# Windowed attention ahead of a mixture of experts: 24 units in one order, scores on row halves, GpSimd normalises every half

## What is computed

```python
scores = (q @ k.T) / sqrt(64)                 # 4 batches, 8 heads, 576 tokens, 64 wide
mask_plain = (rel >= 0) & (rel < 32)          # heads 0 to 3
mask_dil = (rel >= 0) & (rel < 128) & (rel % 4 == 0)   # heads 4 to 7
attn = softmax(where(mask, scores, -1e9))
x = (attn @ v) as [2304 tokens, 512]
x = gate * expert(x)     # one of 8 experts per token, 512 -> 1024 -> 512, ReLU
out = softplus(x @ w_in) @ w_out              # 512 -> 2048 -> 512
```

## Time and profile before

| | us |
|---|---|
| median of 3 runs (813.33 to 814.98) | 814.34 |
| the profiled execution | 813.36 |
| its span, first to last instruction | 811.6 |

### The profile page before, as it was taken

How to read it: one execution, slowest core, us unless ns; L and a number is a source line. 1 busy time by engine, 2 the same in 40 slices (tenths; PEclk the granted TensorE clock), 3 DMA queues, 4 the chain that set the end, 5 groups by cost and what they waited for, 6 DMA issues and landing times.

```text
span 811.6 us, 14035 instructions
## 1 busy us (share of the span) xinstructions
PE 762.9 (94%) x4658; PEld 688.8 (85%) x4659; DVE 446.1 (55%) x910; ACT 398.4 (49%) x1014; POOL 235.2 (29%) x218
## 2 busy tenths in 40 slices
PE   5999996399999999999899999999999999999996
PEld 3667665289999999999899999999999989999995
DVE  8985986864665577767663343343334343334332
ACT  3995894034553566655563453353344344335332
POOL 6220220544666559777830010010010001001001
PEclk9999998589999999999999999999999999999999
DMA  9677202354654666775400010000000000001000
GB/s 247 182 186 271 115 0 117 90 166 152 215 176 136 200 206 192 232 217 181 132 26 1 1 39 0 0 39 0 0 26 13 0 0 39 0 0 39 0 0 39
DMA packets 27258, 74.55 MB, mean 92 GB/s; under 512 B 4112, under 2 KB 12320, under 8 KB 26720
## 3 DMA queue, kind: packets, MB, share of 16 engines
q1 hardware_dynamic: 20624, 53.52, 21.1%
q0 software_dynamic: 5744, 16.02, 6.7%
q10 hardware_dynamic: 864, 4.72, 1.5%
HBM read 64.79 MB, written 9.45 MB: 91 GB/s over the span
## 4 chain that ended last, share of the span: by engine, by line
PE 88%; DVE 7%; issue 2%; ACT 2%; POOL 0%; DVEq 0%; ACTq 0%
PE bank L620 13%; PE bank L622 13%; PE bank L621 13%; PE bank L644 8%; PE bank L646 8%; PE bank L642 8%; PE bank L633 4%; PE bank L635 4%; PE bank L634 4%; PE bank L499 4%; PE bank L523 2%; PE bank L536 2%; PE bank L509 2%; PE bank L606 1%; ACT probs L761 1%
## 5 line engine op out<-in xcount | busy, mean ns | idle before, releaser
L1237 DVE SCALAR_TENSOR_TENSOR g_sb<-bank,soft 128x384 f32<-128x384 f32 x96 | 53.6, 558 | 235.0 <-ACT soft L908 235.0
L904 ACT ACTIVATE soft<-bank 128x384 f32<-128x384 f32 x96 | 47.3, 492 | 208.7 <-PE bank L622 208.7
L471 POOL DMA_INDIRECT out<-y_sb,out_rows_i x18 | 17.5, 971 | 374.9 <-ACT y_sb L915 371.2
L1099 DVE TENSOR_TENSOR w_lo<-raw,w_hi 128x1024 fp32r<-128x1024 f32 x68 | 93.6, 1378 | 50.5 <-ACT w_hi L824 50.4
L620 PE MATMUL bank<-x_parts,w_hi 128*128 (+1 forms) x352 | 111.8, 318 | 3.7 <-DVE w_lo L1099 2.5
L622 PE MATMUL bank<-x_parts,w_lo 128*128 (+1 forms) x352 | 110.9, 315 | 0.0
L621 PE MATMUL bank<-x_parts,w_hi 128*128 (+1 forms) x352 | 110.8, 315 | 0.0
L824 ACT ACTIVATE w_hi<-raw 128x1024 fp32r<-128x1024 f32 x68 | 71.8, 1058 | 50.4 <-PE bank L635 49.6
L406 POOL TENSOR_SCALAR xs_sb<-landing,row_scale 128x256 f32<-128x256 f32 x48 | 64.3, 1348 | 65.8 <-PE bank L606 65.7
L633 PE MATMUL bank<-h_hi,w_hi 128*128 128x384 f32 (+3 forms) x256 | 80.7, 315 | 1.9 <-DVE h_lo L1119 1.9
L761 ACT ACTIVATE probs<-bank,neg_max 96x128 f32<-96x128 f32 x192 | 67.4, 366 | 22.5 <-DVE neg_max L950 22.5
(11 more groups left out here) (201 smaller groups left out, 1776.8 us busy)
## 6 DMA issues: line engine op xcount, KB each, us to landing
raw<-we SPq DMA_DIRECT2D x64, 512.0 KB, 3.5
x_tokens<-x_sb ACTq DMA_DIRECT2D x6, 768.0 KB, 5.1
v_sb<-vw SPq DMA_DIRECT2D x4, 1024.0 KB, 13.6
raw_m<-wm POOLq DMA_DIRECT2D x8, 512.0 KB, 5.2
raw<-wm SPq DMA_DIRECT2D x8, 512.0 KB, 3.6
q_sb<-qT SPq DMA_DIRECT2D x4, 768.0 KB, 9.1
k_sb<-kT SPq DMA_DIRECT2D x8, 384.0 KB, 11.4
v_sb<-vw SPq DMA_DIRECT2D x4, 512.0 KB, 4.7
```

Of the source, the lines that this page charges most:

```text
L1099: nc.vector.tensor_tensor(w_lo[:, r, :], raw[:, r, :], w_hi[:, r, :].bitcast(F32), ALU.subtract).then_inc(w_lo_done, 1)
```

## The change

One stream over all 24 units replaces the two turns; no counters, no turn boundary.

- **Scores on row halves.** A unit's eight heads are scored by eight matmuls of 64 rows and 128 columns. The even heads of the pairs (rows 0 to 63, `par` 0) go to one bank, the odd ones (rows 64 to 127, `par` 1) to the other, in turn. `k_sb` loses its zeros and their memsets, and a key load is one transfer. A bank now holds two plain and two dilated heads.
- **GpSimd normalises both halves** of each unit, one after the other, after one pair of small VectorE operations for the unit (`inverses`).
- **VectorE copies both transposed halves**; ScalarE none.
- **Token tiles between units.** Tiles 0 to 12 are done in units 8 to 11, 14 to 18 and 20 to 23, tiles 13 to 17 after the last unit.
- **Constants.** VectorE clears the masks and spreads the two large index tables from small ones; GpSimd loses those fills. Stores of tiles use three semaphores in turn.

```diff
-        k_sb = [sb(early, f"k_sb{s}", [P, PAIRS, 2, S]) for s in range(2)]
+        k_sb = [sb(early, f"k_sb{s}", [P, PAIRS, S]) for s in range(2)]
...
+        TILE_OF_UNIT = {}
+        for b_, tiles in enumerate((range(0, 4), range(4, 9), range(9, 13))):
+            for n_, g_ in enumerate(tiles):
+                TILE_OF_UNIT[UNITS * (b_ + 1) + 2 + n_] = g_
+        LATE_TILES = range(13, NT)
...
-                for par in range(2):
-                    r = slice(D * par, D * (par + 1))
-                    sp.dma_start(k_sb[m][r, :, par, lo:hi], kT[b][r, :, lo:hi]).then_inc(loaded, 16)
+                sp.dma_start(k_sb[m][:, :, lo:hi], kT[b][:, :, lo:hi]).then_inc(loaded, 16)
...
+            for n in range(2 * ALL_UNITS):
+                c = n % BANKS
+                pool.wait_ge(inv_ready, n // 2 + 1)
+                nc.gpsimd.tensor_tensor(probs[:, c, :, :], probs[:, c, :, :],
+                                        inv_sum[:, c, :].unsqueeze(2).to_broadcast([QT, HEADS, KEYS]), ALU.mult
+                                        ).then_inc(normed[n % 2], 1)
...
+            def scores(u):
...
+                if i == 2:
+                    pe.wait_ge(rest_loaded[m], 48 * (b // 2 + 1))
...
+                for par in range(2):
+                    if u > 1:
+                        pe.wait_ge(exps_done, 2 * (u - 2) + par + 1)
+                    if g is not None:
+                        pe.wait_ge(x_copied_dve if par else x_copied_act, g + 1)
+                    nc.tensor.matmul(banks[par][0:QT, :], identb[:, :], mask, start=True, stop=False,
+                                     skip_group_check=True)
+                for c in range(HEADS):
+                    for par in range(2):
+                        r = slice(D * par, D * (par + 1))
+                        last = nc.tensor.matmul(banks[par][0:QT, KEYS * c:KEYS * (c + 1)],
+                                                q_sb[m][r, c, q0:q0 + QT], k_sb[m][r, c, k0:k0 + KEYS],
+                                                start=False, stop=(c == HEADS - 1), skip_group_check=True)
+                        if c == HEADS - 1:
+                            last.then_inc(scores_done, 1)
...
+            for u in range(ALL_UNITS):
+                g = TILE_OF_UNIT.get(u)
+                if g is not None:
...
+                    pe.wait_ge(exps_done, 2 * u + 2)
+                    token_tile(g)
+                elif u + 2 < ALL_UNITS:
+                    scores(u + 2)
+                if u:
+                    values(u - 1)
+                for par in range(2):
+                    transposes(2 * u + par)
+                if g is not None and u + 2 < ALL_UNITS:
+                    scores(u + 2)
+            values(ALL_UNITS - 1)
+            for g in LATE_TILES:
+                pe.wait_ge(x_copied_act, g - 1)
+                pe.wait_ge(x_copied_dve, g - 1)
+                token_tile(g)
...
+            for u in range(ALL_UNITS):
+                g = TILE_OF_UNIT.get(u)
+                if u + 1 < ALL_UNITS:
+                    exps(2 * u + 2)
+                if g is not None:
+                    x_copy(g)
+                if u + 1 < ALL_UNITS:
+                    exps(2 * u + 3)
+                if u:
+                    dilated_tokens(u - 1)
+                if g is not None and g % TILES_STORED == TILES_STORED - 1:
+                    x_store(g)
...
-                for par in range(2):
-                    nc.vector.memset(k_sb[s][D * par:D * (par + 1), :, 1 - par, :], 0.0).then_inc(k_zeroed[s], 1)
...
+            def inverses(u):
+                pair = slice(2 * (u % 2), 2 * (u % 2) + 2)
+                dve.wait_ge(exps_done, 2 * u + 2)
+                nc.vector.tensor_scalar(sum_eps[:, pair, :], row_sum[:, pair, :], 1e-9, None, ALU.add
+                                        ).then_inc(sums_ready, 1)
+                dve.wait_ge(sums_ready, u + 1)
+                nc.vector.reciprocal(inv_sum[:, pair, :], sum_eps[:, pair, :]).then_inc(inv_ready, 1)
...
+            for u in range(ALL_UNITS):
+                g = TILE_OF_UNIT.get(u)
+                more = u + 2 < ALL_UNITS
+                inverses(u)
+                if g is not None:
+                    x_copy(g)
+                elif more:
+                    for par in range(2):
+                        maxima(2 * (u + 2) + par)
+                if u:
+                    plain_tokens(u - 1)
+                for par in range(2):
+                    copies(2 * u + par)
+                if g is not None and more:
+                    for par in range(2):
+                        maxima(2 * (u + 2) + par)
```

More of the change, by code:

```diff
@@ L226, in build @@
         sizes_ready = sem("sizes_ready")
+        x_stored = [sem(f"x_stored{n}") for n in range(3)]
         raw_loaded = [sem(f"raw_loaded{r}") for r in range(RING)]
@@ L481, in _ @@
         def _(pe):
[L483 to L510, removed]
-                last.then_inc(transposes_done, 1)
-            def values(turn, n):
-                half, j = n % 2, n // 2
-                b, i = j // UNITS, j % UNITS
-                pe.wait_ge(pt_copied[half], turn * TURN + (j + 1 + PT_CREDIT))
-                pe.wait_ge(out_copied_to_x[half], turn * TURN + (j - 1 + OUT_CREDIT))
-                if half == 0 and i == 0:
-                    pe.wait_ge(first_values_loaded[b], turn * 16 + 16)
-                for h in range(HEADS):
-                    r, c = h % 2, 2 * QT * (j % 2) + QT * (h // 2)
-                    last = nc.tensor.matmul(o_ps[half][D * r:D * (r + 1), c:c + QT],
-                                            v_sb[b][:, i, HEADS * half + h, :], probsT[:, n % 2, h, :],
-                                            start=True, stop=True, skip_group_check=True)
-                last.then_inc(values_done, 1)
@@ new lines, in transposes, with values @@
+            def transposes(n):
+                u, par = n // 2, n % 2
+                pe.wait_ge(normed[par], u + 1)
+                if u:
+                    pe.wait_ge(pt_copied[par], u)
+                for c in range(HEADS):
+                    last = nc.tensor.transpose(pt_ps[par][:, QT * c:QT * (c + 1)], probs[:, n % BANKS, c, :],
+                                               ident[0:QT, 0:QT])
+                last.then_inc(transposes_done, 1)
+            def values(u):
+                b, i = u // UNITS, u % UNITS
+                for par in range(2):
+                    pe.wait_ge(pt_copied[par], u + 1)
+                if i == 0:
+                    pe.wait_ge(first_values_loaded[b % 2], 16 * (b // 2 + 1))
+                for c in range(HEADS):
+                    half, place = c // 2, 2 * QT * (u % 2) + QT * (c % 2)
+                    if u and c % 2 == 0:
+                        pe.wait_ge(out_copied_to_x[half], u)
+                    for par in range(2):
+                        last = nc.tensor.matmul(o_ps[half][D * par:D * (par + 1), place:place + QT],
+                                                v_sb[b % 2][:, i, 2 * c + par, :], probsT[:, par, c, :],
+                                                start=True, stop=True, skip_group_check=True)
+                    if c % 2:
+                        last.then_inc(values_done, 1)
@@ L535, in token_tile @@
+            def token_tile(g):
+                pair = pair_of_tile(g)
+                for half in range(2):
+                    pe.wait_ge(out_copied_to_x[half], units_behind(g))
+                t = g % TILES_TURN
                 for k in range(KC):
-                    last = nc.tensor.matmul(x_ps[t % 2][k // 2][:, TW * (k % 2):TW * (k % 2 + 1)],
+                    last = nc.tensor.matmul(x_ps[pair][k // 2][:, TW * (k % 2):TW * (k % 2 + 1)],
                                             xT_sb[:, k, P * t:P * (t + 1)], id_wg[:, k, :], start=True, stop=True,
@@ L1008, in _ @@
+            plain_tokens(ALL_UNITS - 1)
+            for g in LATE_TILES:
+                x_copy(g)
             steps = [0]
```

295 lines of the change are left out of this document (119 added, 176 removed).

## The result

The changed kernel took **828.14 us** in the median of four runs (825.36 to 830.81), against 814.39 (813.33 to 814.98) for the kernel before: a ratio of 1.017, with an interval of 1.013 to 1.021. The forecast was 822.7, with 812 to 838 as the range and 0.84 on slower. The profiled execution took 827.52, with a span of 825.8; before it was 813.36, with 811.6.

A forecast was written before the change was run, and what follows sets the result against it. The attention was to pass from TensorE's chain to a wait loop over GpSimd, TensorE and VectorE: start 21.4, eleven units at 6.28, eleven at 3.74, then the tail, ending at 142.9, 8.4 later. Forecast 822.7 us, range 812 to 838.

The forecast's parts named there:

- rivals 2 and 3: Scores: row halves don't overlap, 837.7 us, chance 0.07; or weight loads bound the row halves, 831.5 us, chance 0.05.
- Where the loss would be, and its sign: Attention ends 8.4 us later (142.9 against 134.5), the later part unchanged; slower overall had chance 0.84.
- The tile units: Units with a token tile: multiplications, transposes, scores and maxima stand in a row, 6.28 us each, for eleven intervals.
- The plain units: Units without a token tile: a wait loop over GpSimd, TensorE and VectorE, 3.74 us each, for eleven intervals.
- two maxima at 0.82 (40.72 to 41.53) 1.64: VectorE's two maxima in the wait loop take 1.64 us, read from one place in the earlier trace.
- The start: Before the steady units: unit 1's inverses start at 21.4 us, after loads landing at 17.2; constants and clears hidden.
- The tail: After unit 23's inverses at 131.6: 3.67 to its last copy, values 0.81, result copy 0.7, five tiles at 1.07, copy 0.7.
- The sum: Start, units and tail together put the attention's last token copy at 142.9 us, 8.4 later than before.
- 1 (GpSimd's pairs quicker): GpSimd's paired multiplications at 0.69 us instead of 1.04 make the kernel faster, 810.6 us; chance 0.12.
- 4, the clock: TensorE's clock drops to 1.2 GHz throughout the attention, 29 us more, 852 us; chance 0.04.
- the longest idle stretch is about 1 us, so 0.04: TensorE's pauses in the attention reach only about 1 us, so the clock drop got chance 0.04.
- with 3.07 busy of 4 us it was granted 1.00: An earlier window where TensorE, busy 3.07 of 4 us, kept full clock; compared with 4.1 of 6.3 in tile units.

The follow-up runs named there:

- the order experiment: Changed kernel with, in tile units only, scores and maxima of the next unit but one put ahead of the transposes and their copies: 818.76 us, ratio 1.002.
- The first experiment: Changed kernel with VectorE's `neg_max` in the form that also sums into an accumulator, the sum read by nothing: 829.78 us, ratio 1.016.

## Why the prediction was right, and where its terms were off

The direction, the place of the loss and the chain came out as forecast; the size did not (14.05 for 8.4). That 828.14 stayed in 812 to 838 owes something to luck: the upper part of that range was there for rivals 2 and 3, and neither came true. What filled it were two terms that the prediction had at nothing.

**Where the loss would be, and its sign.** Right. The attention left TensorE's chain for a loop of waits over GpSimd and VectorE; the rest of the kernel is unchanged (677.3 against 677.1).

**The tile units.** 6.28 each was forecast. Eight of eleven took 6.2, the chain with the added matmuls shows the same links, and the order experiment took exactly the row of waits away (5.22). The three others, at half clock, took 4.0 more than three at 6.21: eleven take 72.3 instead of 69.1.

**The plain units.** 3.74 each was forecast, 41.1 for eleven; they took 44.5. The first took 4.92, mostly at half clock (+1.2). The other ten took 3.64 six times and 4.43 four times, +2.1. The step that failed is "two maxima at 0.82 (40.72 to 41.53) 1.64". It was read at a place that could not show the effect, and put into a loop in which GpSimd is busy half of the time. At 41.44, where its `neg_max` starts, GpSimd's multiplication has 0.15 left; at 17.51, in the timeline, one has 0.48 left. The kernel before, there and at the place that was read:

```profile
17.51 0.50 DVE L950 TENSOR_SCALAR neg_max<-row_max 96x4 f32<-96x4 f32 x1
...
40.55 1.04 POOL L384 TENSOR_TENSOR probs<-probs,inv_sum 96x512 f32<-96x512 f32 x1 [2.94 <-DVE inv_sum L958]
```

With the multiplication of the earlier trace rows (16.95 to 17.99) the first row ends at 18.01, as the one at 35.33 does with its pair. The first experiment showed the cause. Two GpSimd multiplications in a row were expected at 2 x 1.04 and took 2.04; the prediction had asked whether VectorE's work slows GpSimd, and not whether GpSimd's slows VectorE. The groups of the kernel before hinted at it too: the mean of `neg_max` over its 48 was 288 ns, against 0.17 when alone (two at the start, 1.68 and 1.09 long beside GpSimd's index fills, are part of that mean). The Trainium skill has the rule, in "SBUF — State Buffer", section "Who interferes with whom": of VectorE and GpSimd, whoever issues first holds the shared pair of ports for the whole instruction; a `tensor_scalar` can need it, its form that writes out the accumulator cannot, a `tensor_reduce` never does. The traces agree in all three (0.83 and 0.153 for `neg_max`; `row_max` at 0.68 under GpSimd or not), and with its case of a VectorE instruction with two inputs from SBUF too (1.54 for 1.04, though 0.14 less than a wait for all of VectorE's multiplication would give). With it, an estimate from the 4.43 and 3.64 of the plain units, the sum would have come 2 us later.

**The start.** 21.4 was forecast for the inverses of unit 1; it was 20.64. The loads landed 2 us earlier (15.04 for 17.23), and half clock took part of that back (sixteen score records in 2.03 at 16.06). Hidden as said: spreading the tables, the clears, the stores (the first maximum starts at 8.97, released by the scores). The tail took 11.07 instead of 11.3.

**The sum.** 142.9 became 148.51. +5.6 is: start -0.8; plain units +3.3, of which the port 2.1; tile units +3.3, of which the clock +4.0; tail -0.2. Without port conflict and, but for the start, without half clock, it is 142.26.

**The rivals.** 1 (GpSimd's pairs quicker) is refuted by 2.04 for two. 2 and 3 are refuted by the 1.10 of sixteen records. 4, the clock, was given 0.04 and half came true: not at 1.2 GHz throughout, but in four stretches that cost 5 us together. The step that failed is "the longest idle stretch is about 1 us, so 0.04", and ahead of it "with 3.07 busy of 4 us it was granted 1.00". In the changed kernel TensorE was busy 20.75 of 26.4 us in the tile units, and lost the clock within them, where the waits are not longer than 1.20 us. The row that was used, 76 to 80 us, is four microseconds of the refill behind the turn, with one pause of 0.93; it was put on a stretch in which such pauses come in every unit, and that they cost nothing there was not shown by it.

**What was only argued.** What in a tile unit makes the clock fall in one and not in the next is not shown; that filling its waits keeps it up is, in two profiled runs. Why what follows the attention took 677.3 in one profile and up to 681.1 in others is not shown either.

## What to carry to other kernels

A multiplication moved to an engine with spare time is hidden only if no one waits for it in the same round; draw the loop over the in-order streams before counting busy time, and give the result one round of lag if it closes such a loop. Take the duration of a small VectorE operation from places where GpSimd is as busy as it will be, and compare its mean over all its occurrences with its shortest. Once TensorE waits in places where it was solid, look for half clock in windows and test it with work that nothing uses before any other cause is named.

## What the runs showed of the hardware that was not expected

- A VectorE operation on 96 x 4 elements took 0.17 alone and up to 0.94 under a GpSimd multiplication; in the form that sums into an accumulator it took 0.15 each time, with a second instruction of 0.08 behind it. The other way round GpSimd's multiplication grew from 1.04 to 1.54 when it started 0.05 behind a VectorE multiplication of 0.69.
- The granted clock fell to 0.50 for 3.4 us at a time, in three to five tile units of a run, in other units each time, with TensorE busy 20.75 of 26.4 us over four such units and waits of at most 1.2 us. With sixteen matmuls in one of these waits of each tile unit it stayed at 1.00 in all 22 tile units of two profiled runs. The half clock of the first 19 to 24 us, ahead of these matmuls, was there with and without them.
- Scores on two row halves run as fully side by side as values on two column halves: sixteen records of 128 columns, each with 96 columns of weights of its own, in 0.86, the change of shape and a hop (1.10 together).
